# Attention with a gated and a mixing layer on one core: every part of the probabilities split in two, the division moved behind the product

## The reference

```
q_rot, k_rot = rotate(q), rotate(k)      # x1*cos - x2*sin, x1*sin + x2*cos
scores = q_rot @ k_rot.T / 8 - max
attn = exp(scores); attn = attn / (attn.sum(-1) + 1e-9)
x = attn @ v                             # then x[:, heads*64+d]
k = relu((mu_k*x + (1-mu_k)*x_prev) @ w_k); r = sigmoid((... mu_r ...) @ w_r)
x = r * (k*k @ w_v)                      # then the mixing over tokens and channels
```

## Time and profile before

| | us |
|---|---|
| median of 3 runs | 1056.86 |
| the 3 runs | 1062.91, 1056.86, 1056.76 |
| the profiled execution | 1058.53 |
| its span, first to last instruction | 1056.7 |
| busy: TensorE, VectorE, ScalarE, GpSimd | 998.6, 668.1, 567.1, 314.9 |
| mean granted TensorE clock | 0.992 |

### The profile page before, as it was taken

How to read it: one execution, slowest core, us unless ns; L and a number is a source line. 1 busy time by engine, 2 the same in 40 slices (tenths; PEclk the granted TensorE clock), 3 DMA queues, 4 the chain that set the end, 5 groups by cost and what they waited for, 6 DMA issues and landing times.

```text
span 1056.7 us, 21205 instructions
## 1 busy us (share of the span) xinstructions
PE 998.6 (94%) x7040; PEld 930.8 (88%) x7040; DVE 668.1 (63%) x1330; ACT 567.1 (54%) x1344; POOL 314.9 (30%) x317
## 2 busy tenths in 40 slices
PE   5888999998999998999999999999999999999997
PEld 4777777777888878999999999788999999999997
DVE  6999999999999997978666775455221221221220
ACT  4888999988999996444444442642131131121120
POOL 5777877877676721100000000342000000000000
PEclk9999999999999999999999999999999999999999
DMA  3122222222112101100000000130000000000000
GB/s 90 48 58 59 55 55 60 61 59 56 35 40 47 35 14 48 61 1 0 0 0 0 0 0 0 60 119 2 1 24 23 1 23 22 0 22 20 3 22 22
DMA packets 70078, 32.90 MB, mean 31 GB/s; under 512 B 62496, under 2 KB 63392, under 8 KB 70048
## 3 DMA queue, kind: packets, MB, share of 16 engines
q1 hardware_dynamic: 69760, 32.20, 11.4%
q10 hardware_dynamic: 288, 0.33, 0.1%
HBM read 27.79 MB, written 4.72 MB: 31 GB/s over the span
## 4 chain that ended last, share of the span: by engine, by line
PE 62%; DVE 18%; issue 11%; ACT 7%; DVEq 1%; DMA 0%; ACTq 0%; SPq 0%
PE psum L559 19%; PE psum L561 18%; PE psum L560 18%; DVE row_stats L974 4%; DVE pT_lo L991 3%; ACT probs L756 3%; DVE row_stats L997 2%; DVE probs L1004 2%; DVE pT_hi L991 2%; PE psum L530 1%; DVE qT L955 1%; ACT pT_hi L769 1%; PE psum L544 1%; DVE xT L1013 1%; PE psum L649 1%
## 5 line engine op out<-in xcount | busy, mean ns | idle before, releaser
L932 ACT ACTIVATE h_hi<-psum 128x288 fp32r<-128x288 f32 x96 | 39.5, 411 | 245.8 <-PE psum L561 245.8
L530 PE MATMUL psum<-ident,probs 128*128 128x128 f32 x800 | 138.4, 285 | 30.4 <-ACT pT_hi L769 12.9
L530 PEld LDWEIGHTS psum<-ident,probs 128*128 128x128 f32 x800 | 92.4, 142 | 55.7 <-ACT pT_hi L769 17.3
L974 DVE TENSOR_REDUCE row_stats<-psum 128x1 f32<-128x576 f32 (+1 forms) x160 | 119.9, 749 | 8.0 <-ACT probs L756 4.0
L1178 DVE SCALAR_TENSOR_TENSOR h_lo<-psum,h_hi 128x288 fp32r<-128x288 f32 x96 | 44.0, 458 | 125.8 <-ACT h_hi L932 125.8
L756 ACT ACTIVATE probs<-psum,row_stats 128x576 f32<-128x576 f32 (+1 forms) x160 | 118.8, 743 | 6.2 <-DVE row_stats L974 4.4
L559 PE MATMUL psum<-u_hi,wc_hi 128*128 128x288 f32 x384 | 114.3, 298 | 0.2 <-DVEq L1172 0.2
L559 PE MATMUL psum<-h_hi,wc_hi 128*128 128x288 f32 x384 | 113.7, 296 | 0.0
L560 PE MATMUL psum<-u_lo,wc_hi 128*128 128x288 f32 x384 | 113.3, 295 | 0.0
L560 PE MATMUL psum<-h_lo,wc_hi 128*128 128x288 f32 x384 | 113.3, 295 | 0.0
L561 PE MATMUL psum<-h_hi,wc_lo 128*128 128x288 f32 x384 | 112.9, 294 | 0.0
(11 more groups left out here) (137 smaller groups left out, 2940.1 us busy)
## 6 DMA issues: line engine op xcount, KB each, us to landing
stage_w<-in_moe_w_ch_dram SPq DMA_DIRECT2D x8, 768.0 KB, 4.4
out_dram<-stage_out SPq DMA_DIRECT2D x8, 576.0 KB, 3.7
raw_q<-in_q_dram SPq DMA_DIRECT2D x32, 128.0 KB, 2.2
raw_k<-in_k_dram SPq DMA_DIRECT2D x32, 128.0 KB, 2.3
raw_v<-in_v_dram SPq DMA_DIRECT2D x32, 128.0 KB, 2.1
stage_w<-in_moe_w_k_dram SPq DMA_DIRECT2D x4, 512.0 KB, 3.8
stage_w<-in_moe_w_v_dram SPq DMA_DIRECT2D x4, 512.0 KB, 3.5
raw_v<-in_v_dram SPq DMA_DIRECT2D x64, 16.0 KB, 2.0
```

Source lines behind the costliest of these rows:

```text
L530: ins = t.transpose(bank[:, at:at + P], probs[i][:, tile, at_key:at_key + P], ident[:, :])
L974: d_.tensor_reduce(neg_max[0:m, at:at + 1], score_banks[at][0:m, :, 0:HALF], AX.XY, ALU.max, negate=True).then_inc(maxed, 1)
```

## The change

- **All units split.** `WHOLE` is empty: units 1, 4 and 5 get lo parts on VectorE (L1, L4, L5), and products with hi and lo in float32r in place of float32.
- **Division behind the product.** N0 to N4 go. The transposes wait for the exponentials alone. One `invert` per head, at the end of the next slot, over all 5 sums. SyncE writes the 128 x 5 inverses to DRAM in rows (`sums_out`), reads them back spread over 64 partitions (`sums_back`), and GpSimd multiplies the finished `xT` of two heads by them (`scale_x`, 128 x 576, one per round).
- **q in pairs.** q is rotated once, not doubled; one transpose turns two q tiles (3, and 1 for k's tail, in P0; 4 for k in the last P). ScalarE and VectorE take q in two instructions, odd and even tiles. GpSimd multiplies q and k by the tables together (128 x 640), then adds. P0 waits for q and k.
- **Weights.** They are loaded straight to where the lo parts will stand (`w1_raw` lies over `w1_lo`), without a staging buffer, and split in 20 pieces of 512, one per round and the rest at the end. Piece n of round `it` waits for the loads of rounds 0 to `it` (`w1_in`). In SyncE's order the load stands behind the sums' write, the next values and the sums' reading back.
- **Orders.** New texts for three engines; v stands behind E1 and H4 on ScalarE.

```diff
-    WHOLE = (1, 4, 5)
+    WHOLE = ()
...
-    ACT_ORDER = steps("H0 H1 E0 N4 H2 P0 v0 H3 E1 O0 H4 P1 H5 E2 H6 H7 N1 P2 E3 O1 E4")
...
+    ORDER = steps("S0 T0 T1 P0 S1 T2 V0 T3 S2 T4 V1 V2 T5 S3 T6 P1 T7 V3 S4 V4 V6 V5 V7")
+    ACT_ORDER = steps("H0 H1 P0 E0 P1 H2 P2 H3 E1 H4 v0 O0 H5 E2 H6 H7 P3 E3 O1 E4")
+    DVE_ORDER = steps("M0 L0 L1 M1 L2 P0 L3 M2 L4 P1 P2 L5 O0 M3 L6 L7 P3 M4 I0 O1")
...
+        PIECE = N_WV * UNIT // HALF_UNITS
...
+        w1_raw = nc.alloc_sbuf_tensor_at("w1_raw", [P, N_WV * UNIT], F32, offset=base + N_WV * UNIT * FLOAT)
...
+            a = by_cos[:, j, :, h * half:(h + 1) * half]
+            b = by_sin[:, j, :, (1 - h) * half:(2 - h) * half]
+            if j == 0:
+                return rot[:, 0:NT, h * half:(h + 1) * half], a, b
...
-            def load_w1(w, it, first, tiles, again=True):
-                if again:
-                    sp.wait_ge(w_lo, it)
+            def load_w1(w, it, first, tiles):
                 src = w[bass.ds(it * (tiles * P) + (-first * tiles * P), tiles * P), :].rearrange("(t p) n -> p t n", p=P)
-                sp.dma_start(stage_w1[:, :].rearrange("p (t n) -> p t n", t=tiles), src).then_inc(w1_in, 16)
-            def load_pair(it, w=None, first=0, tiles=1, again=True):
-                it_is_zero = isinstance(it, int) and it == 0
-                for i in range(2):
-                    sp.wait_ge(k_roped, upto(it, i, 1, 1))
-                    load_qk(it * 2 + (2 + i), i)
-                    if not (it_is_zero and i == 0):
-                        sp.wait_ge(v_used, upto(it, i, 1, 0))
-                        load_v(it * 2 + (1 + i), 1 - i)
-                    if w is not None and i == 0:
-                        load_w1(w, it, first, tiles, again)
+                sp.dma_start(w1_raw[:, bass.ds(it * UNIT, UNIT)].rearrange("p (t n) -> p t n", t=tiles), src).then_inc(w1_in, 16)
+            def sums_out(it, kk):
+                sp.wait_ge(sum_inv, upto(it, kk, 1, 1))
+                sp.dma_start(sum_rows[bass.ds(it * 2 + kk, 1), :].rearrange("o (t p) -> p (o t)", p=P),
+                             rsums[:, kk % 2, :], allow_slow_non_contiguous=True).then_inc(sums_stored, 16)
+            def sums_back(it, kk, first=False):
+                i = kk % 2
+                sp.wait_ge(sums_stored, it * 32 + (16 * kk + 16))
+                if i == 0 and not first:
+                    sp.wait_ge(x_scaled, it)
+                sp.dma_start(rb[i * D:i * D + D, :], sum_rows[bass.ds(it * 2 + kk, 1), 0:S].to_broadcast([D, S])).then_inc(rb_in, 16)
+            def next_v(it, kk):
+                sp.wait_ge(v_lo_ready, upto(it, kk, 1, 0))
+                sp.wait_ge(v_used, upto(it, kk, 1, 0))
+                load_v(it * 2 + (kk + 1), (kk + 1) % 2)
+            def next_qk(it, kk):
+                sp.wait_ge(k_roped, upto(it, kk, 1, 3))
+                load_qk(it * 2 + (kk + 4), kk % 2)
+            def slots(it, w=None, first=0, tiles=1, more=True, start=False):
+                if not start:
+                    sums_out(it, -1)
+                    next_v(it, 0)
+                    sums_back(it, -1)
+                if w is not None:
+                    load_w1(w, it, first, tiles)
+                if more:
+                    next_qk(it, 0)
+                sums_out(it, 0)
+                next_v(it, 1)
+                sums_back(it, 0, first=start)
+                if more:
+                    next_qk(it, 1)
...
+                    pool.wait_ge(prep_turned, upto(it, kk - 2, 2, 2))
+                    pool.wait_ge(k_roped, upto(it, kk, 1, 0))
+                g.tensor_tensor(times_cos[:, :, :, :], raw_qk[i][:, :, :, :], both(cos), ALU.mult).then_inc(rope_step, 1)
+                g.tensor_tensor(times_sin[:, :, :, :], raw_qk[i][:, :, :, :], both(sin), ALU.mult).then_inc(rope_step, 1)
+                pool.wait_ge(rope_step, upto(it, kk - 1, 2, 2))
+                for j, (rot, done) in enumerate(((rot_q[i], q_roped), (rot_k[i], k_roped))):
+                    g.tensor_tensor(*rope_half(rot, times_cos, times_sin, j, 0), ALU.subtract)
+                    g.tensor_tensor(*rope_half(rot, times_cos, times_sin, j, 1), ALU.add).then_inc(done, 1)
...
+            def piece(it):
+                return bass.ds(it * PIECE, PIECE)
+            def split_w1_hi(it, n):
+                pool.wait_ge(w1_in, n * 16)
+                g.tensor_copy(w1_hi[:, piece(it)], w1_raw[:, piece(it)]).then_inc(w_hi, 1)
             def split_w1_lo(it):
-                pool.wait_ge(w_hi, it + 1)
-                g.tensor_tensor(w1_lo[:, w1_at(it)], stage_w1[:, :], w1_hi[:, w1_at(it)], ALU.subtract).then_inc(w_lo, 1)
+                g.tensor_tensor(w1_lo[:, piece(it)], w1_raw[:, piece(it)], w1_hi[:, piece(it)], ALU.subtract).then_inc(w_lo, 1)
+            def scale_x(p):
+                pool.wait_ge(span_out, p * 4 + 4)
+                pool.wait_ge(rb_in, p * 32 + 32)
+                at = bass.ds(p * COLS + 1, S)
+                g.tensor_tensor(xT[:, at], xT[:, at], rb[:, :], ALU.mult).then_inc(x_scaled, 1)
...
+            def slots(it, n, scaling):
+                split_v(it, 0, 0)
+                rotate(it, 0, 2, False)
+                split_w1_hi(it, n)
+                pool.wait_ge(w_hi, it + 1)
+                split_v(it, 1, 1)
+                split_w1_lo(it)
+                rotate(it, 1, 3, False)
+                if scaling:
+                    scale_x(it - 1)
+            slots(0, 1, False)
+            with pool.Fori(1, N_WV) as it:
+                slots(it, it + 1, True)
             with pool.Fori(N_WV, HEADS // 2 - 1) as it:
-                for i in range(2):
-                    split_v(it, i, i)
-                    rotate(it, i, i + 2, False)
-            for i in range(2):
-                split_v(HEADS // 2 - 1, i, i)
+                slots(it, N_WV, True)
+            last = HEADS // 2 - 1
+            split_v(last, 0, 0)
+            for n in range(last, HALF_UNITS):
+                split_w1_hi(n, N_WV)
+                pool.wait_ge(w_hi, n + 1)
+                split_w1_lo(n)
+                if n == last:
+                    split_v(last, 1, 1)
+                if n == last + 2:
+                    scale_x(last - 1)
+            scale_x(last)
...
+                        pe.wait_ge(q_roped, upto(it, kk, 1, 1))
+                        pe.wait_ge(k_roped, upto(it, kk, 1, 1))
+                        pe.wait_ge(prep_lo, upto(it, kk, 4, 0))
+                    for p in range(PAIRS):
+                        t.transpose(prep_bank[:, p * P:(p + 1) * P], rot_q[i][:, 2 * p:2 * p + 2, :].rearrange("p a d -> p (a d)"), ident[:, :])
+                    ins = t.transpose(prep_bank[:, PAIRS * P:PAIRS * P + P], rot_k[i][:, FULL, :, :].rearrange("p a d -> p (a d)"), ident[:, :])
...
-                    pe.wait_ge(normed_act, upto(it, kk, ACT_TILES, len([x for x in BY_ACT if x < hi])))
-                    pe.wait_ge(normed_dve, upto(it, kk, NT - ACT_TILES, len([x for x in range(hi) if x not in BY_ACT])))
+                    pe.wait_ge(expd, upto(it, kk, NT, hi))
...
+            def invert(it, i, kk, first):
+                dve.wait_ge(expd, upto(it, kk, NT, NT))
+                if not first:
+                    dve.wait_ge(sums_stored, it * 32 + (16 * kk - 16))
+                d_.tensor_scalar(rsums[:, i, :], sums[:, i, :], 1e-9, None, ALU.add).then_inc(sum_plus, 1)
+                dve.wait_ge(sum_plus, upto(it, kk, 1, 1))
+                d_.reciprocal(rsums[:, i, :], rsums[:, i, :]).then_inc(sum_inv, 1)
```

287 lines of the change are left out of this document (133 added, 154 removed).

## The result

| | before | after |
|---|---|---|
| median (4 runs each) | 1056.81 us | 1228.05 us |
| range of the runs | 1055.77 to 1062.91 | 1227.50 to 1228.19 |
| span of the profiled execution | 1056.7 | 1225.5 |
| mean granted TensorE clock | 0.992 | 0.918 |

The ratio is 1.160, with a 95% interval of 1.157 to 1.164. The prediction was 1069, with 1081 as the upper end of its range.

A forecast was written before the change was run, and what follows sets the result against it. The loop through GpSimd (23.7 us a round) and, in rounds 1 to 9, the weights' load (25.85) bound attention: +13.5 by head 30, -1 at the last head, +12.5 on 1058.53; median 1069.3, range 1043 to 1081.

The forecast's parts named there:

- The weights' load in this loop: Rounds 1 to 9: GpSimd waits for weights loaded behind the inverses' trip, so rounds take 25.85 us; the write counted as covered.
- Rival 3: The small write of inverses is slow, 1.6 us beyond cover in nine rounds: +14, about 1083 us; chance 0.10.
- Rival 1: The weights' load hides and only the loop through GpSimd holds, rounds of 23.7 us: median about 1050 us; chance 0.18.
- M4 of head 2: The 64-row maximum marking the end of head 2's slot: forecast at 46.2 us, against 48.67 before.
- P0 to the end of v: The loop's leg over the four transposes and ScalarE's steps up to the values' copy: 4.4 us, bounds 4.1 and 4.8.
- round by the loop: Two slots bound by P0, v, GpSimd's split and rotation, P0: 11.23 plus 12.46, 23.7 us at the least.
- round with the weights' load: Rounds 1 to 9, where GpSimd waits for weights ahead of its second split: 25.85 us from P0 to the next but one.
- round by VectorE alone: What VectorE's work allows for two slots: 22.1 us, or 23.1 with its waits for GpSimd.
- VectorE's sum of -0.15 a slot: Divisions and an inversion go, L1, L4, L5 and smaller pieces come: -0.15 of 11.27 us a slot on VectorE.
- the stall of its addition on GpSimd: VectorE waits where it meets a GpSimd instruction: 0 to 1.5 us a slot, 0.5 taken as the mean.
- Edits at nothing: Edits priced at zero: scale_x's 1.4 us in GpSimd's wait for v, late weight pieces, the mixing's wait, q and k loads.
- Rival 2: The loop through GpSimd hides too, by some 0.6 us a round; VectorE holds with 23.1: about 1042 us; chance 0.13.

The follow-up runs named there:

- e15: The kernel before with a read of 640 single numbers, into a tile nobody uses, added ahead of the values of heads 2 to 30: 1072.8 us.
- e8: The kernel before with a write of 640 single numbers side by side, read by nobody, added ahead of the values of heads 2 to 30: 1240.31 us.
- e4: The changed kernel with the write of the inverses issued from ScalarE's queue, behind H1 of the next slot: 1231.6 us.
- e17: The kernel before with a write of 128 single numbers, 64 bytes apart in DRAM, added ahead of each head's values: 1073.99 us.
- e1: The changed kernel without the inverses' write and reading back, a constant 0.004 in their place (other output): 1080.49 us, ratio 1.021.
- e2: The changed kernel with the inverses written as 128 pieces of 20 bytes and read by GpSimd in transposed order: 1098.94 us, ratio 1.039.
- e5: e1 with the weights' load ahead of all that waits in SyncE's round: 1069.54 us, ratio 1.011.
- e6: e5 with the values issued first on SyncE and v moved from behind H4 to behind H0 on ScalarE: 1030.29 us, ratio 0.974.
- e7: The changed kernel with inverses written in 20-byte pieces, weights and values issued ahead of them, v behind H0: 1029.08 us, ratio 0.973.
- e11: The kernel before with a write of 128 single numbers side by side, read by nobody, added ahead of each head's values: 1157.94 us.
- e14: The kernel before with a write of 128 pieces of 8 bytes, side by side, added ahead of each head's values: 1084.57 us.
- e12: The kernel before with a write of 128 pieces of 20 bytes added ahead of each head's values: 1074.7 us.
- e13: The kernel before with a write of 128 single numbers, 512 bytes apart in DRAM, added ahead of each head's values: 1074.86 us.
- e18: The kernel before with a write of 640 single numbers, 512 bytes apart in DRAM, added ahead of each head's values: 1077.88 us.

## Why the prediction was wrong, by its steps

**The step that failed** is the pricing of the small write in "The weights' load in this loop": it took the read of mu, 2.3 us to landing, as the nearest row, called the write covered by the 2.5 us of issues, and kept 1.6 us as the other end. The neighbour was wrong in kind. A read of 640 singles does cost 2.1 us (e15), so mu was no exception; a write of them into neighbouring addresses costs 9.06 us in the slot above, and 9.3 as the median of the 22 of 32 writes with all landing records. It also reaches further than the step had it: the step priced it only for the weights of rounds 1 to 9, while it holds every head's values as well, in all rounds (e8: 158 us of waits in the kernel before).

**Rival 3** named the mechanism, a slow write of singles, with 0.10. Its place and size were off: "nine rounds more by 1.6". The stall of SyncE on the landing, its own sign, is there: 6.7 us without an issue behind the values (307.57 to 314.26), 150.3 us in all. It counted only what SyncE does late and left out that later transfers, though issued, land late too, from either queue (e4). The doubt on the page of the Trainium skill, DMA: Bandwidth & Descriptors, section Specifications, pointed the right way for this write. But by its rule all pieces under 512 bytes should suffer, and 128 single numbers 64 bytes apart landed in 1.4 us (e17): the measurement narrows the late landing to pieces that lie side by side. Whether reading and modifying is what makes it late, no run here shows.

**Rival 1** was priced against itself in one place: the load would have to be early by 25.85 - 23.7 = 2.15 us for the loop alone to hold, not by 1.4.

**The other terms**, read where the write is out of the way (e1, e2 and e5):

| term | forecast | measured |
|---|---|---|
| M4 of head 2 | 46.2 | 48.5 (e1), 48.8 (e5) |
| P0 to the end of v | 4.4 (4.1 to 4.8) | 4.65 |
| round by the loop | 23.7 | 24.4 (e5), 24.5 (e1) |
| round with the weights' load | 25.85 | 26.1 (e1), 27.6 (e2) |
| round by VectorE alone | 22.1, 23.1 with stalls | 22.1 (e6, e7) |

- The loop was right: TensorE waits at P0 in nearly every slot, and moving v and its load forward removes it (e5 to e6, 39 us; ScalarE waits for the values' load in neither). Its 0.7 us a round too little is 0.25 in each of the two slots on ScalarE's leg, by the slot shown under e5, and the rest in the slot with the piece of weights.
- The weights' load was right in mechanism: GpSimd waits 5.1 us a round for it in e1, about 5 forecast. With a fast trip, which is what the term was a sum of, it is 1.8 us short; e1 has no trip, whose two issues are 1.1 us of the sum, so 24.75 would be the forecast for it, and 26.1 was measured. Some 1.3 of the 1.8 is thus there without any trip, and was not taken apart; the rest is the landing and the reading back. A fast write would have given head 30 at 420.07 against the 397.4 forecast: 2.5 from the start, 9 times 1.8, and 5 times 0.8. So even with the write priced at 1.5 us the forecast of 1069 would have been 30 us low (e2, 1098.94), 23 of them up to head 30 and the rest behind it.
- VectorE's sum of -0.15 a slot holds. So does the stall of its addition on GpSimd, for which 0.5 was taken: the addition took 0.15 us where it met nothing, and 610 ns on the mean in e1, so the stall is 0.46. In the changed kernel, whose GpSimd stands idle more, the mean is 313 ns; in e6 it is 230:

```profile
L1077 DVE TENSOR_SCALAR rsums<-sums 128x5 f32<-128x5 f32 x32 | 19.5, 610 | 0.0
```

```profile
L1078 DVE TENSOR_SCALAR rsums<-sums 128x5 f32<-128x5 f32 x32 | 10.0, 313 | 0.4 <-ACT probs L837 0.4
```

- Edits at nothing: `scale_x` took its 1.4 us in GpSimd's wait for v, as forecast. The stage behind attention stayed: TensorE is busy 281.4 of the last 289.0 us, 281.5 before.
- Left out altogether: the granted clock. The forecast took all products at full clock, and attention ran at 0.82 of it. How much of the 171 us that is wasn't taken apart, since no run here has the stalls without the lower clock. An estimate from two windows: up to the 64-row maximum of head 31 TensorE is busy 371.7 us in the changed kernel (559.70 us long, clock 0.83) and 333.0 in e1 (415.04 us long, clock 0.95), for the same products. So some 39 of the 145 us between them are products that took longer, and the rest is idle time.

**Rival 2**, both loops hidden, isn't what the changed kernel does once its write is fast (e2: TensorE waits at P0 in 30 slots). Other orders had to make it so: e6 and e7 take 1030 and 1029 us, where 1042 was forecast for that state.

## What to carry to other kernels

Price a DMA by a row of the same direction and the same layout in DRAM; before writing a column of single numbers in transposed order, let each partition write what it holds as one piece, and transpose where the data is read. Look at what stands behind a slow transfer in every queue, not only at who waits for its landing. Where a loop runs through several engines, ask for the one step whose place in an order closes it: here v on ScalarE, with its load, worth 39 us.

## What the runs showed of the hardware that was not expected

- Writes from SBUF to DRAM, 128 pieces each, issue to landing (medians): 4 bytes side by side, 8.1 us (e11); 8 bytes side by side, 3.8 (e14); 20 bytes side by side, 1.4 (e12); 4 bytes with 64 or 512 bytes from one to the next, 1.4 (e17, e13). Of 640 pieces of 4 bytes: 10.0 us side by side (e8), 2.7 when 512 bytes apart (e18). Read, 640 side by side: 2.1 us (e15).
- The slow write isn't long on the DMA engines. Its packets of 4 bytes take 8.5 ns on the mean in e8 and are through within 0.5 us in the slot looked at; the landing comes 9.7 us after the issue.
- A slow write holds transfers issued behind it on the same queue (ScalarE waited up to 7.3 us for values in e8) and on another queue (e4: values landed after 8.7 to 11.8 us instead of 3.0 to 3.3). By what means wasn't settled.
- In the changed kernel the weights are issued after the write has landed, and still take 5.2 to 5.9 us to landing, against 4.0 in e2 with the same order and the fast write. Why is open.
- Why the landing is late for pieces side by side stays open too: no run here shows the addresses at work.
